# First group of a fused recurrence and two-layer MLP kernel on one Trainium2 core: all first-layer weight loads queued ahead of the decays of group 2, two buffers for the range-check sums, other slots for sums and scans

## The chip, the core and the metric

One core of a Trainium2 chip runs the whole kernel. The metric is the device time of one execution in microseconds. Three runs of the kernel before gave 985.7, 987.65 and 989.75 us, median 987.65. The trace is of one more execution.

## The reference

```
for t in range(768):                        # B=4, H=8, D=48: y is (B,H,S,D)
    y[:, :, t] = r[t] @ (state + outer(u * k[t], v[t]))
    state = w[t][..., None] * state + outer(k[t], v[t])
x = y transposed to (3072 tokens, 384)
h = x @ w_in                                # 384 -> 2048
g = where(h >= 1, h, where(h <= -1, 0, (h + 1)**2 / 4))
x = g @ w_out                               # 2048 -> 384
g2 = x @ w_gate;  v2 = x @ w_val            # 384 -> 1536 each
out = (g2 * sigmoid(g2) * v2) @ w_out2      # 1536 -> 384
```

All in float32. The kernel computes each float32 product as three products of a high and a low part (`hi*hi`, `lo*hi`, `hi*lo`).

## The kernel before

**Tiling.** The 3,072 tokens are eight groups of 384 tokens, a group is three windows of 128. `phase1` goes over the groups and, in each, over 16 slots `j` of the first MLP; `phase2` does the same for the second MLP. In slot `j` TensorE runs `tile_in(j+2)` (nine matmuls of 128x384, L1142) and `tile_out(j)` (nine, L1170). ScalarE and VectorE make the activation between the two: ScalarE `knee` (L761, L763), VectorE `knee` (L1004), ScalarE `hi` (L754, rounds to the high part), VectorE `lo` (L997, the low part). VectorE's slot `j` begins with `lo(j+1)` and `knee(j+2)`.

**The recurrence** of group g+1 is computed in the slots of group g. VectorE scans the decays `w` backwards and forwards (`suffix_scan` L907 and L910, `prefix_scan` L917; both together are `scan_window`), scales `k` and `r` (`scale_window`, L929 and L932), sums the products of one token (`diag_sum`, L937), decays the state (L958), masks the attention tile (L973), adds up the state (L985) and the output of a window (L989), and splits the transposed output (L992). TensorE's pieces of it are called fills: KT (L1185), AT (L1193), ST (L1202), Y (L1210, L1215) and XT (L1221). A fill needs a bank of PSUM that an earlier fill's readers have given back: AT of window 1 needs the banks of Y and ST of window 0, so it waits for L989 and L985. `WIN_SLOTS` puts the fills into slots 3, 5, 6, 8, 9, 11 and 12. GpSimd makes the token products (`diag_products`, L658 and L661) and, from the sums, the values (`diag_values`, L668).

**The first group is special.** Its own recurrence runs before slot 0 with nothing beside it. And in it the weights of the first MLP arrive: 32 chunks `c` of 192 KB, even ones of `w_in`, odd ones of `w_out`. The queue of SyncE loads chunk c into slot c % 13 of a ring, once both parts of chunk c - 13 are made (`load_w1`). ScalarE makes the high part (`w1_hi`, L699), two chunks in each slot; the low part is made by GpSimd (L645) for three chunks of four and by VectorE (`w1_lo`, L1033) for every fourth: 3, 7, 11 up to 31. `tile_in(j)` needs chunk 2j and `tile_out(j)` chunk 2j+1.

**What sets the order.** Every engine and the queue of SyncE go in program order, which is written out by hand. Tables say in which slot of group 0 VectorE and ScalarE do what for group 1: `CHECK_FIRST`, `SCAN_FIRST`, `SCALE_FIRST`, `DIAG_FIRST`, `LO_FIRST`. `PRODUCTS_AT` and `VALUES_AT` say after which chunk GpSimd makes the products and values of a window of group 1. SyncE issues `load_w(2, w)`, the decays of group 2, ahead of the last five weight chunks (27 to 31); each waits until VectorE has scaled the same window of group 1 (`scaled`, L932), because the tile is reused.

**The range check.** ScalarE's `check_w` (L715) sums, over each window, how far `w` lies outside of the range for which the fast scans hold, into the six columns of `beyond`; VectorE's `sum_w` (L943) adds them to `bad`. With one `beyond` the check of the next group may begin only when `sum_w` of the group before is done. A slow exact version behind `If(flagged > 0)` is not taken here.

Of the kernel before, what the change touches and what calls it, by code (L numbers as in the profile page):

```python
# [24 lines left out]
F32 = mybir.dt.float32  # L25
F32R = mybir.dt.float32r
U32 = mybir.dt.uint32
ALU = mybir.AluOpType
# [8 lines left out]
NW = 3  # L37
# [3 lines left out]
PR = 64 + D  # L41
KT = DM // P
J1, J2 = FF1 // P, FF2 // P
# [4 lines left out]
RING = 13  # L48
# [23 lines left out]
OPS_CHECK = 2 * NW  # L72
# [13 lines left out]
CHECK_FIRST = {0: 1, 2: 2}  # L86
SCAN_FIRST = {1: 1, 4: 2}
SCALE_FIRST = {0: 0, 2: 1, 7: 2}
DIAG_FIRST = {2: 0, 4: 1, 6: 2}


DVE_LO = 4
LO_FIRST = {0: 7, 1: 11, 3: 15, 4: 19, 6: 23, 8: 27, 10: 31}
PRODUCTS_AT = {8: 0, 13: 1, 20: 2}
VALUES_AT = {12: 0, 18: 1, 25: 2}


def first(g):
    return isinstance(g, int) and g == 0
# [6 lines left out]
def fill_no(g, kind, w, n=0):  # L106
    return fills(g).index((kind, w, n))


def build_program(nc, w_d, kr_d, tok_d, u_d, cst_d, w1i_d, w1o_d, w2g_d, w2v_d,  # L110
                  w2o_d, rs_d, ks_d, vs_d, ws_d, us_d, out_d, x2_d, ys_d):
    ctx = ExitStack()
    with ctx:
        at = [nc.sbuf_base + (-nc.sbuf_base) % 32]

        def place(name, shape, dt, offset=None):

            size = 2 if dt == mybir.dt.bfloat16 else 4
            for n in shape[1:]:
                size *= n  # L120
            if offset is None:
                offset = at[0]
                at[0] += (size + 31) // 32 * 32
            assert offset + size <= nc.sbuf_usable_end, (name, offset + size)
            return nc.alloc_sbuf_tensor_at(name, shape, dt, offset=offset), offset + size
# [11 lines left out]


        checked, _ = place("w_checked", [PR, NPAIR * WIN], mybir.dt.bfloat16)
        beyond, _ = place("w_beyond", [PR, OPS_CHECK], F32)  # L140
        bad, _ = place("w_bad", [PR, OPS_CHECK + 1], F32)
        ones, _ = place("ones", [PR, 1], F32)

# [359 lines left out]
        def _(e):  # L503
# [13 lines left out]
            def load_w1(n):  # L517

                for c in range(chunk[0], min(chunk[0] + n, 2 * J1)):
                    if c >= RING:  # L520
                        wait(whi, c - RING + 1)
                        wait_lo(wait, c - RING)
                    src = (w1i_d if c % 2 == 0 else w1o_d)[c // 2]
                    e.dma_start(chunk_raw(c), src).then_inc(raw[c % RING], 16)
                chunk[0] += n
# [13 lines left out]
            def load_tok(g, w):  # L539

                if g > 0:
                    wait(fill, (g - 1) * NF + fill_no(g - 1, "ST", w) + 1)
                    wait(y_out, (g - 1) * NW + w + 1)
                e.dma_start(tok[:, w, :, :], tok_d[g, w]).then_inc(ld["tok", w], 16)
# [8 lines left out]
            load_w(0, 2)  # L553
            load_kr(0, 2)
            load_tok(0, 1)
            load_w1(1)
            load_tok(0, 2)
            load_w1(3)
            for w in range(NW):
                load_w(1, w)  # L560
            load_w1(RING - 4)
            for w in range(NW):
                load_kr(1, w)
                load_tok(1, w)
            load_w1(14)
            for w in range(NW):
                load_w(2, w)
            load_w1(2 * J1)

            def half(g, after_next):  # L570

# [123 lines left out]
        def _(e):  # L695
# [5 lines left out]
            def check_w(g, w):  # L701

                if w == 0:
                    if first(g):
                        e.wait_ge(tables, 1)
                    else:
                        e.wait_ge(w_sum, g + 1)
                e.wait_ge(ld["w", w], (g + 1) * 16)
                src = tokens_of(w_at, w)[:, :, 1:]
                junk = checked[:, :].rearrange("q (p t) -> q p t", t=WIN)  # L710
                for k, (scale, bias) in enumerate(((-1.0, W_LOW), (1.0, -W_HIGH))):
                    m = 2 * w + k
                    if not (first(g) and m == 0):
                        e.wait_ge(w_seen, g * OPS_CHECK + m)
                    e.activation(junk, src, ACT.Relu, bias=bias, scale=scale,  # L715
                                 accum_out=beyond[:, m:m + 1]).then_inc(w_seen, 1)

            def decay_first(w):

# [67 lines left out]
            drain(0, fill_no(0, "ST", 0), 0)  # L787
            decay_first(1)
            drain(0, fill_no(0, "KT", 1), 0)
            done = [0]  # L790

            def more_hi(n):
# [10 lines left out]
            drain(0, fill_no(0, "XT", 1), 0)  # L803
            more_hi(8)
            drain(0, fill_no(0, "XT", 2), 0)
            check_w(1, 0)
            more_hi(11)
            knee(0, 0)
            hi(1, 0, 0)
# [88 lines left out]
        def _(e):  # L898
# [41 lines left out]
            def sum_w(g):  # L940
                e.wait_ge(w_seen, (g + 1) * OPS_CHECK)
                e.wait_ge(w_sum, g + 1)
                e.tensor_tensor(bad[:, 0:OPS_CHECK], bad[:, 0:OPS_CHECK], beyond[:, :], ALU.add).then_inc(w_sum, 1)  # L943

            def decay_state(g, w, parity):

# [82 lines left out]
            def w1_lo(c):  # L1029
                t = w1i if c % 2 == 0 else w1o  # L1030
                e.wait_ge(whi, c + 1)
                e.wait_ge(raw[c % RING], 16 * (c // RING + 1))
                e.tensor_tensor(t[1][:, c // 2, :], chunk_raw(c), t[0][:, c // 2, :].bitcast(F32),  # L1033
                                ALU.subtract).then_inc(wlo_d, 1)
# [22 lines left out]
            drain(0, fill_no(0, "XT", 1), 0)  # L1057
            drain(0, fill_no(0, "XT", 2), 0)
            drain(0, fill_no(0, "ST", 2), 0)
            suffix_scan(1, 0)  # L1060
            w1_lo(3)
            prefix_scan(1, 0)
            knee(0, 0)
            lo(1, 0, 0)
            knee(0, 1)

            def nxt(g, j, J_):
                return (g, j) if j < J_ else (g + 1, j - J_)
# [289 lines left out]
```

## Time and profile before

| | |
|---|---|
| three runs, median | 987.65 us (985.7 to 989.75) |
| the profiled execution, its own time | 987.91 us |
| its span, first to last instruction | 986.0 us |
| TensorE busy | 960.7 us, 97% |
| VectorE, ScalarE, GpSimd busy | 522.1, 404.3, 149.6 us |
| mean granted TensorE clock | 0.996 |
| group 0, slot 0 begins at | 35.9 us |
| group 0, slot 15 ends near | 107 us |

The span counts from the first to the last instruction, and what lies around it in this execution is 1.9 us. An engine's busy time counts an instruction from its start to its end, waiting for a shared resource included. An idle time stands in front of the instruction that ended it, with what released it.

### The profile page before, as it was taken

The numbers are of one execution on the slowest core, as the hardware profiler recorded it, in microseconds if no ns is written. First come the engines' busy times: TensorE is split into PE (matmuls) and PEld (weight loads), VectorE is DVE, ScalarE is ACT, GpSimd is POOL, SyncE is SP. The second block draws the span as 40 slices with busy tenths as digits, with TensorE's granted clock in tenths as the row PEclk, the third lists the DMA queues.
The fourth block names the chain that finished last, engine by engine and source line by source line (L and its number), as shares of the span: only waits on it lengthen the run. The fifth ranks groups of instructions, "written<-read, shape, count | busy, mean of one in ns | idle before, by whom it ended". The sixth has DMA issues, their size and how long they took to land.

```text
span 986.0 us, 17455 instructions
## 1 busy us (share of the span) xinstructions
PE 960.7 (97%) x6874; PEld 942.0 (96%) x6874; DVE 522.1 (53%) x913; ACT 404.3 (41%) x849; POOL 149.6 (15%) x146
## 2 busy tenths in 40 slices
PE   5898999999999999999999999999999999999997
PEld 4888999999999999999999999999999999999997
DVE  8895757657576665665434434434343343344332
ACT  5855546445464454544565322222222222222221
POOL 6582120211202102020263300000000000000000
PEclk9998999999999999999999999999999999999999
DMA  7916131321313222100332201010100001010000
GB/s 249 279 34 178 44 96 47 93 77 54 96 44 95 58 73 81 59 25 1 121 105 89 73 1 49 1 49 2 48 0 15 33 0 48 0 48 0 25 1 26
DMA packets 23204, 59.52 MB, mean 60 GB/s; under 512 B 2656, under 2 KB 11616, under 8 KB 23136
## 3 DMA queue, kind: packets, MB, share of 16 engines
q1 hardware_dynamic: 23136, 58.59, 19.0%
q8 instruction: 46, 0.75, 0.3%
q14 instruction: 22, 0.18, 0.1%
HBM read 49.14 MB, written 9.44 MB: 59 GB/s over the span
## 4 chain that ended last, share of the span: by engine, by line
PE 91%; DVE 4%; issue 1%; DMA 1%; ACT 1%; SPq 0%; DVEq 0%; ACTq 0%
PE bank L1142 48%; PE bank L1170 34%; PE bank L1193 3%; PE bank L1215 2%; PE bank L1210 2%; PE bank L1185 1%; PE bank L1221 1%; PE bank L1202 1%; DVE glo L997 1%; DVE suf L907 1%; DVE k_r_by_channel L929 1%; DMA ring<-in_w_gate 1%; DVE gate L1004 1%; DVE k_r_by_channel L932 0%; DVE state_decayed L958 0%
## 5 line engine op out<-in xcount | busy, mean ns | idle before, releaser
L997 DVE TENSOR_TENSOR glo<-gate,ghi 128x384 fp32r<-128x384 f32 x224 | 134.6, 601 | 114.6 <-ACT ghi L754 112.2
L754 ACT ACTIVATE ghi<-gate 128x384 fp32r<-128x384 f32 x224 | 117.2, 523 | 189.9 <-DVE gate L1016 95.4
L1014 DVE TENSOR_TENSOR gate<-bank,gate 128x384 f32<-128x384 f32 x96 | 53.5, 558 | 215.0 <-ACT gate L873 215.0
L1142 PE MATMUL bank<-xhi,w2gv_ahi 128*128 128x384 f32 x480 | 161.3, 336 | 0.0
L1142 PE MATMUL bank<-xlo,w2gv_ahi 128*128 128x384 f32 x480 | 161.3, 336 | 0.0
L1142 PE MATMUL bank<-xhi,w2gv_alo 128*128 128x384 f32 x480 | 161.3, 336 | 0.0
L873 ACT ACTIVATE gate<-bank 128x384 f32<-128x384 f32 x96 | 47.2, 492 | 227.7 <-PE bank L1142 227.7
L1170 PE MATMUL bank<-ghi,w1ohi 128*128 128x384 f32 x384 | 134.6, 350 | 0.3 <-DVE glo L997 0.3
L1142 PE MATMUL bank<-xhi,w1ihi 128*128 128x384 f32 x384 | 129.5, 337 | 4.2 <-DVE gate L1004 1.5
L1170 PE MATMUL bank<-glo,w1ohi 128*128 128x384 f32 x384 | 129.7, 338 | 0.0
L1170 PE MATMUL bank<-ghi,w1olo 128*128 128x384 f32 x384 | 129.6, 337 | 0.0
L1142 PE MATMUL bank<-xhi,w1ilo 128*128 128x384 f32 x384 | 129.2, 336 | 0.0
L1142 PE MATMUL bank<-xlo,w1ihi 128*128 128x384 f32 x384 | 129.1, 336 | 0.0
L1004 DVE SCALAR_TENSOR_TENSOR gate<-bank,gate 128x384 f32<-128x384 f32 x128 | 71.1, 556 | 106.2 <-ACT gate L763 106.1
L761 ACT ACTIVATE gate<-bank 128x384 f32<-128x384 f32 x128 | 62.7, 490 | 90.2 <-PE bank L1142 90.2
L1170 PE MATMUL bank<-ghi,w2ohi 128*128 128x384 f32 x288 | 96.8, 336 | 0.0
L1170 PE MATMUL bank<-ghi,w2olo 128*128 128x384 f32 x288 | 96.8, 336 | 0.0
L1170 PE MATMUL bank<-glo,w2ohi 128*128 128x384 f32 x288 | 96.8, 336 | 0.0
L1142 PEld LDWEIGHTS bank<-xhi,w2gv_ahi 128*128 128x128 f32 x480 | 90.2, 188 | 0.0
L1142 PEld LDWEIGHTS bank<-xlo,w2gv_ahi 128*128 128x128 f32 x480 | 90.2, 188 | 0.0
L1142 PEld LDWEIGHTS bank<-xhi,w2gv_alo 128*128 128x128 f32 x480 | 90.2, 188 | 0.0
L1142 PEld LDWEIGHTS bank<-xhi,w1ihi 128*128 128x128 f32 x384 | 72.3, 188 | 5.0 <-issue 3.2
(90 smaller groups left out, 1530.7 us busy)
## 6 DMA issues: line engine op xcount, KB each, us to landing
r_k_v_by_token<-in_rkv_token SPq DMA_DIRECT2D x24, 576.0 KB, 4.9
k_r_by_channel<-in_kr_channel SPq DMA_DIRECT2D x24, 448.0 KB, 3.9
w_by_channel<-in_w_channel SPq DMA_DIRECT2D x24, 226.2 KB, 2.7
x_t<-ring SPq DMA_DIRECT2D x8, 576.0 KB, 3.0
x_raw<-x_t SPq DMA_DIRECT2D x8, 576.0 KB, 4.0
out_t<-ring SPq DMA_DIRECT2D x8, 576.0 KB, 3.1
ring<-in_w_out SPq DMA_DIRECT2D x22, 192.0 KB, 3.3
ring<-in_w_gate SPq DMA_DIRECT2D x12, 192.0 KB, 2.3
```

Source lines behind the costliest of these rows:

```text
L754: e.activation(ghi[j % 2][:, :], gate[j % 2][:, :], ACT.Copy).then_inc(M["hi", ph], 1)
L761: e.activation(q, hid[j % 2][:, 0:T], ACT.Relu, bias=0.5, scale=0.5).then_inc(M["q", 1], 1)
L873: e.activation(gate[j % 2][:, :], hid[j % 2][:, 0:T], ACT.Sigmoid).then_inc(M["q", 2], 1)
L907: e.tensor_tensor_scan(suf[:, w, ::-1], w_at[:, w, :0:-1], last[:, ::-1], 0.0, ALU.mult, ALU.max).then_inc(scan, 1)
L997: e.tensor_tensor(glo[j % 2][:, :], gate[j % 2][:, :], ghi[j % 2][:, :].bitcast(F32), ALU.subtract)\
L1004: e.scalar_tensor_tensor(q, hid[j % 2][:, 0:T], 1.0, q, ALU.max, ALU.min).then_inc(M["g", 1], 1)
L1014: e.tensor_tensor(q, hid[j % 2][:, 0:T], q, ALU.mult).then_inc(M["t", 2], 1)
L1142: m = e.matmul(out, w_of(a, k), x_of(b_, k), start=start and i == 0, stop=stop and i == total - 1)
L1170: m = e.matmul(acc[k][:, 0:T], wo[a][:, j, k * P:(k + 1) * P], gs[b_][:, :], start=(j == 0 and i == 0), stop=(j == J[ph] - 1 and i == 2))
L1193: m = e.matmul(o[:, p * WIN:(p + 1) * WIN], kr[r, w, 0, p, :], kr[r, w, 1, p, :], start=True, stop=True)
L1210: e.matmul(out[t, p * 2 * D:(p + 1) * 2 * D], kr[:, w, 1, p, t], sbar[twin(g, w)][:, p, :], start=(p == 0), stop=False, skip_group_check=True)
L1215: m = e.matmul(out[t, h * D:(h + 1) * D], att[twin(g, w)][h % 2][:, h // 2, t], tok[:, w, 2, h * D:(h + 1) * D], start=(row_start and h == 0),
```

## The change

1. **SyncE's queue, late.** `load_w(2, w)`, w = 0, 1, 2, goes behind all 32 weight chunks; it stood behind chunk 26.
2. **SyncE's queue, early.** `load_w(1, 0)` goes ahead of chunk 0 and of the tokens of window 2, and chunk 4 goes ahead of `load_w(1, 1)`.
3. **Checks.** `beyond` gets two buffers, one for even and one for odd groups, and `check_w(g, 0)` waits only for the sum of group g-2. ScalarE's `check_w(1, 0)` moves from behind XT of window 2 to behind KT of window 1 of group 0.
4. **VectorE.** `w1_lo(3)` goes ahead of `suffix_scan(1, 0)`, and `prefix_scan(1, 0)` behind `knee(0, 1)`. The `diag_sum`s of group 1 go from slots 2, 4, 6 to 0, 3, 5; chunk 15 goes from slot 3 to 2 and chunk 27 from slot 8 to 9.
5. **GpSimd.** Values of windows 0, 1, 2 behind chunks 13, 19, 26 (before 12, 18, 25), products of window 1 behind chunk 14 (before 13).

```diff
-DIAG_FIRST = {2: 0, 4: 1, 6: 2}
+DIAG_FIRST = {0: 0, 3: 1, 5: 2}
-LO_FIRST = {0: 7, 1: 11, 3: 15, 4: 19, 6: 23, 8: 27, 10: 31}
-PRODUCTS_AT = {8: 0, 13: 1, 20: 2}
-VALUES_AT = {12: 0, 18: 1, 25: 2}
+LO_FIRST = {0: 7, 1: 11, 2: 15, 4: 19, 6: 23, 9: 27, 10: 31}
+PRODUCTS_AT = {8: 0, 14: 1, 20: 2}
+VALUES_AT = {13: 0, 19: 1, 26: 2}
...
-        beyond, _ = place("w_beyond", [PR, OPS_CHECK], F32)
+        beyond, _ = place("w_beyond", [PR, 2, OPS_CHECK], F32)
...
             load_tok(0, 1)
+            load_w(1, 0)
             load_w1(1)
             load_tok(0, 2)
-            load_w1(3)
-            for w in range(NW):
+            load_w1(4)
+            for w in range(1, NW):
                 load_w(1, w)
-            load_w1(RING - 4)
+            load_w1(RING - 5)
...
-            load_w1(14)
+            load_w1(2 * J1)
             for w in range(NW):
                 load_w(2, w)
-            load_w1(2 * J1)
...
                 if w == 0:
-                    if first(g):
-                        e.wait_ge(tables, 1)
-                    else:
-                        e.wait_ge(w_sum, g + 1)
+                    e.wait_ge(tables, 1)
+                    if g > 1:
+                        e.wait_ge(w_sum, g)
...
-                                 accum_out=beyond[:, m:m + 1]).then_inc(w_seen, 1)
+                                 accum_out=beyond[:, g % 2, m:m + 1]).then_inc(w_seen, 1)
...
             drain(0, fill_no(0, "KT", 1), 0)
+            check_w(1, 0)
...
             drain(0, fill_no(0, "XT", 2), 0)
-            check_w(1, 0)
             more_hi(11)
...
             drain(0, fill_no(0, "ST", 2), 0)
+            w1_lo(3)
             suffix_scan(1, 0)
-            w1_lo(3)
-            prefix_scan(1, 0)
             knee(0, 0)
             lo(1, 0, 0)
             knee(0, 1)
+            prefix_scan(1, 0)
```

`sum_w` reads `beyond[:, g % 2, :]` accordingly. Where the rows of the order speak of the changed kernel, its line numbers from ScalarE's part on are one lower.

**SyncE, the end of group 0's weight loads; before:**

```order
L524 DMA ring_b<-in_w_out 128x384
L524 DMA ring<-in_w_in 128x384
L531 DMA w_by_channel<-in_w_channel 112x517 x3
L524 DMA ring<-in_w_out 128x384
L524 DMA ring<-in_w_in 128x384
L524 DMA ring<-in_w_out 128x384
```

and changed:

```order
L524 DMA ring<-in_w_out 128x384
L524 DMA ring<-in_w_in 128x384
L524 DMA ring<-in_w_out 128x384
L531 DMA w_by_channel<-in_w_channel 112x517 x3
L537 DMA k_r_by_channel<-in_kr_channel 112x1024
```

The three loads of decays (L531) stood between chunks 26 and 27; now they stand behind chunk 31 and directly ahead of the `k` and `r` of group 2.

**GpSimd, from chunk 9 on, first where the low parts of chunks 12 to 18 and the products and values of group 1 stand** (L645 is a low part, L658 and L661 the products, L668 the values). What is printed is the difference of the two:

```order
 L645 TENSOR_TENSOR w1olo<-ring_b,w1ohi 128x384
 L645 TENSOR_TENSOR w1ilo<-ring_b,w1ihi 128x384 x2
+L645 TENSOR_TENSOR w1olo<-ring,w1ohi 128x384
 L668 TENSOR_TENSOR r_k_v_by_token<-r_k_v_by_token,diag 128x384
-L645 TENSOR_TENSOR w1olo<-ring,w1ohi 128x384
+L645 TENSOR_TENSOR w1ilo<-ring,w1ihi 128x384
 L658 TENSOR_TENSOR r_k_v_by_token<-r_k_v_by_token 128x384
 L661 TENSOR_TENSOR r_k_v_by_token<-r_k_v_by_token,u_rows 128x384
-L645 TENSOR_TENSOR w1ilo<-ring,w1ihi 128x384 x2
+L645 TENSOR_TENSOR w1ilo<-ring,w1ihi 128x384
```

Chunk 13 now goes ahead of the values of window 0, and chunk 14 ahead of the products of window 1.

**VectorE, slots 0 to 3 of group 0; before, from `scale_window(1, 0)` of slot 0 on:**

```order
L929 TENSOR_TENSOR k_r_by_channel<-k_r_by_channel,suf 112x512
L932 TENSOR_TENSOR k_r_by_channel<-k_r_by_channel,w_by_channel 112x512
L1033 TENSOR_TENSOR w1olo<-ring_b,w1ohi 128x384
L997 TENSOR_TENSOR glo_57<-gate_53,ghi_55 128x384
L1004 SCALAR_TENSOR_TENSOR gate_54<-bank,gate_54 128x384
L907 SCALAR_TENSOR_TENSOR suf<-w_by_channel,last_of_segment 112x516
L910 RECIPROCAL scan_seed<-suf 112x4
L917 SCALAR_TENSOR_TENSOR w_by_channel<-w_by_channel,scan_seed 112x516
```

and changed:

```order
L928 TENSOR_TENSOR k_r_by_channel<-k_r_by_channel,suf 112x512
L931 TENSOR_TENSOR k_r_by_channel<-k_r_by_channel,w_by_channel 112x512
L936 TENSOR_REDUCE diag<-r_k_v_by_token 128x8
L1032 TENSOR_TENSOR w1olo<-ring_b,w1ohi 128x384
L996 TENSOR_TENSOR glo_57<-gate_53,ghi_55 128x384
L1003 SCALAR_TENSOR_TENSOR gate_54<-bank,gate_54 128x384
L906 SCALAR_TENSOR_TENSOR suf<-w_by_channel,last_of_segment 112x516
L909 RECIPROCAL scan_seed<-suf 112x4
L916 SCALAR_TENSOR_TENSOR w_by_channel<-w_by_channel,scan_seed 112x516
```

The sum of window 0 (L936) stands two slots earlier, ahead of chunk 7; the rest of the order is kept there.

## Rows read from the trace of the kernel before

**Rows 1.** Waits of TensorE (engine, line, releaser: us in total, times, longest), 0 to 140 us

```profile
PE bank L1193 <- DVE x_by_token L989: 3.8, 2, 3.0
PE bank L1142 <- DVE gate L1004: 1.5, 1, 1.5
PE bank L1142 <- POOL w1ilo L645: 1.4, 1, 1.4
```

**Rows 2.** Busy time by stretch: PE, PEld, DVE, ACT, POOL, then granted clock, DMA share, GB/s

```profile
42.00:49.50 7.50, 7.50 (x55) 7.20 (x54) 7.36 (x14) 7.09 (x18) 0.00 (x0) 1.00 0.80 258
49.50:62.00 12.50, 11.11 (x117) 10.52 (x116) 12.30 (x17) 6.29 (x14) 12.36 (x10) 1.00 0.20 64
75.00:80.00 5.00, 2.47 (x15) 2.15 (x13) 1.39 (x5) 1.81 (x4) 0.69 (x1) 0.97 0.84 240
80.00:85.00 5.00, 4.57 (x25) 4.38 (x26) 3.94 (x8) 2.17 (x6) 0.95 (x2) 0.50 0.96 258
```

**Rows 3.** Timeline of SyncE's queue: start, us, line, transfer

```profile
52.32 22.15 SPq L531 DMA_DIRECT2D w_by_channel<-in_w_channel  x3
```

**Rows 4.** Timelines of ScalarE and VectorE behind that load; in brackets the idle time

```profile
78.10 0.52 ACT L699 ACTIVATE w1ohi<-ring 128x384 fp32r<-128x384 f32 x1 [3.19 <-DMA ring<-in_w_out]
...
79.59 0.73 DVE L985 TENSOR_TENSOR state<-bank,state_decayed 48x192 f32<-48x192 f32 x2
```

**Rows 5.** Timeline of TensorE: first matmuls of `tile_in` 8, 9, 11, 12; AT of windows 1, 2

```profile
61.10 0.34 PE L1142 MATMUL bank<-xhi,w1ihi 128*128 128x384 f32 x1
...
63.71 1.16 PE L1193 MATMUL bank<-k_r_by_channel 48*128 48x128 f32 x16 [0.89 <-DVE x_by_token L989]
...
66.75 0.34 PE L1142 MATMUL bank<-xhi,w1ihi 128*128 128x384 f32 x1
...
75.75 0.34 PE L1142 MATMUL bank<-xhi,w1ihi 128*128 128x384 f32 x1
...
80.43 2.08 PE L1193 MATMUL bank<-k_r_by_channel 48*128 48x128 f32 x16 [2.96 <-DVE x_by_token L989]
...
86.02 0.52 PE L1142 MATMUL bank<-xhi,w1ihi 128*128 128x384 f32 x1
```

**Rows 6.** Timeline of GpSimd: chunk 12, and the values of window 0 that followed

```profile
40.40 1.33 POOL L645 TENSOR_TENSOR w1ilo<-ring_b,w1ihi 128x384 fp32r<-128x384 f32 x1 [1.03 <-ACT w1ihi L699]
49.56 1.01 POOL L668 TENSOR_TENSOR r_k_v_by_token<-r_k_v_by_token,diag 128x384 f32<-128x384 f32 x1 [7.84 <-DVE diag L937]
```

**Rows 7.** VectorE's groups of instructions, 42.1 to 49.5 us: busy us, mean ns

```profile
L997 DVE TENSOR_TENSOR glo<-gate,ghi 128x384 fp32r<-128x384 f32 x3 | 1.6, 549 | 0.0
...
L907 DVE TENSOR_TENSOR_SCAN suf<-w_by_channel,last_of_segment 112x516 f32<-112x516 f32 x1 | 1.2, 1217 | 0.0
...
L1033 DVE TENSOR_TENSOR w1olo<-ring_b,w1ohi 128x384 fp32r<-128x384 f32 x2 | 1.1, 538 | 0.0
```

**Rows 8.** The same groups of VectorE, 49.5 to 62 us

```profile
L997 DVE TENSOR_TENSOR glo<-gate,ghi 128x384 fp32r<-128x384 f32 x3 | 2.7, 900 | 0.0
L958 DVE TENSOR_TENSOR state_decayed<-state,suf 48x192 f32<-48x192 f32 x2 | 2.2, 1113 | 0.0
L1004 DVE SCALAR_TENSOR_TENSOR gate<-bank,gate 128x384 f32<-128x384 f32 x3 | 1.6, 547 | 0.0
L1033 DVE TENSOR_TENSOR w1olo<-ring,w1ohi 128x384 fp32r<-128x384 f32 x2 | 1.6, 787 | 0.0
L907 DVE TENSOR_TENSOR_SCAN suf<-w_by_channel,last_of_segment 112x516 f32<-112x516 f32 x1 | 1.6, 1569 | 0.0
```

**Rows 9.** Timeline of VectorE: `lo(2)`, `lo(6)`, state of window 0, decay of window 2

```profile
42.67 0.55 DVE L997 TENSOR_TENSOR glo<-gate,ghi 128x384 fp32r<-128x384 f32 x1
...
60.41 1.18 DVE L997 TENSOR_TENSOR glo<-gate,ghi 128x384 fp32r<-128x384 f32 x1
...
62.88 0.73 DVE L985 TENSOR_TENSOR state<-bank,state_decayed 48x192 f32<-48x192 f32 x2
...
81.42 0.73 DVE L958 TENSOR_TENSOR state_decayed<-state,suf 48x192 f32<-48x192 f32 x2
```

More of the change, by code:

```diff
@@ L942, in sum_w @@
                 e.wait_ge(w_sum, g + 1)
-                e.tensor_tensor(bad[:, 0:OPS_CHECK], bad[:, 0:OPS_CHECK], beyond[:, :], ALU.add).then_inc(w_sum, 1)
+                e.tensor_tensor(bad[:, 0:OPS_CHECK], bad[:, 0:OPS_CHECK], beyond[:, g % 2, :], ALU.add).then_inc(w_sum, 1)
             def decay_state(g, w, parity):
```

## The prediction

> **What bounds the kernel now.** The first view is the list of TensorE's waits together with the busy time by stretch. TensorE is busy for 97% of the span, and the waits of any size are in group 0 and at the two ends. In slots 0 to 15 of group 0 it waited four times: twice for the bank of L1193 (0.9 and 3.0 us), 1.5 us for `knee(0, 0)` of VectorE, and 1.4 us for the low part of chunk 14 by GpSimd [rows 1]. The reader should see that the largest wait is one alone, and that the stretch around it is also the only one in which the granted clock is 0.50 [rows 2].
>
> The second view is the timeline of the engines around that wait. SyncE's queue was at the decays of group 2 from 52.32 to 74.47 us, because the last of these waits for L932 of window 2, and chunk 27 stands behind it [rows 3]. ScalarE had come to chunk 27 and idled 3.19 us for its landing, VectorE stood behind ScalarE's high part, and only then came the drains of window 1 (L989, L985), whose banks AT of window 2 needs [rows 4]. TensorE resumed at 80.43 us, after 2.96 us, and its sixteen matmuls of AT then took 2.08 us where those of window 1 took 1.16 [rows 5].
>
> The third view, VectorE's busy time, says what comes next. In 42 to 62 us VectorE was busy for 19.66 of 20 us, and TensorE's wait at 63.7 us ended with VectorE's L985 of window 0 (62.88 + 0.73 us) [rows 2, 5, 9]. So up to the load stall the pace is set by VectorE, with TensorE close behind. And VectorE's time is not all its own: from 42 to 49.5 us GpSimd did nothing and `lo` took 549 ns, a low part of a chunk 538, a suffix scan 1,217; from 49.5 to 62 us GpSimd was busy 12.36 of 12.5 us and the same took 900, 787 and 1,569, the decays of a window 2.2 us for the pair against 0.73 alone. `knee`, which reads a bank, took 547 either way [rows 2, 6 to 9]. I read this as the two engines taking turns at something that instructions with two SBUF inputs need.
>
> **Part 1, the late loads (the gain).** With all 32 chunks ahead of L531, chunk 27 waits only for the low part of chunk 14, and chunk 31 for that of 18, all of which exist before 61 us; the queue was idle then. The stall of ScalarE and VectorE goes. Its price is read as a whole: from `tile_in(11)` to `tile_in(12)` TensorE took 86.02 - 75.75 = 10.27 us. The same work (AT, XT, `tile_out`, `tile_in`) took 66.75 - 61.10 = 5.65 us two windows earlier, 0.89 of it waiting and 0.17 the last matmul running out, so 4.6 without a wait [rows 5]. The stall cost 5.7 us: 3.0 of waiting and 2.7 of half clock. Behind it L531 comes to wait for window 2 of group 1 as before, and the decays, `k` and `r` of group 2 go out right then, where five chunks stood ahead of them: nothing becomes later.
>
> **Part 2, the early loads and the moved check: nothing.** `load_w(1, 0)` and the chunks behind it wait for L932 of window 0, but there transfers are queued up behind one another, so the order of bytes counts and not the moment of issue. 226 KB more ahead of the tokens of window 2 is 0.9 us at the 258 GB/s of another full stretch [rows 2], and GpSimd comes to those tokens late. ScalarE's check falls into an idle stretch ahead of KT of window 2. If that cover were gone, its 1.5 us would stand ahead of that drain; where it was, ScalarE now is free 1.4 us earlier, ahead of `knee(0, 0)`.
>
> **Part 3, the prefix scan and the two first waits: nothing in the end.** `knee(0, 0)` no longer stands behind a scan, and TensorE's 1.5 us go. But what was moved (1.2 us of scan) and the sum of window 0 (0.5 us) are now ahead of slot 1, so VectorE reaches `lo(2)` at about 42.6 us, as before (42.67) [rows 1, 9]. The wait for chunk 14 (1.4 us) goes too, since GpSimd no longer idles ahead of it. Both gains are swallowed at the next point where TensorE catches up with VectorE.
>
> **Part 4, GpSimd's turns (the loss).** Before, GpSimd idled 7.84 us for the sum of window 0 [rows 6], and these were VectorE's undisturbed slots. Now the sum is done ahead of slot 1 and GpSimd runs on: chunk 13, values, chunk 14, products (two), chunks 16, 17, 18, of which none ran before 49.5 us before. In slots 1 to 3 VectorE has its longest strings of two-input instructions (two scans, chunk 11, `lo(3)`; then L929, L932, chunk 15, `lo(4)`), and behind each of them a waiting GpSimd gets its turn. I count up to `lo(6)`. Before, from 42.67 to 60.41 + 1.18 = 61.59 us, VectorE took 18.9 us. Of these the excess over undisturbed was 3 x 0.35 (`lo`) + 1.5 (decays) + 2 x 0.25 (chunks) + 2 x 0.35 (scans) = 3.75 us, for 9 instructions of GpSimd: 0.42 each [rows 7 to 9]. Own work is 15.2 us, now 14.7 without the sum. Against it stand 14 instructions of GpSimd (5 more: chunks 20, 21, 22 and the two products of window 2). A turn costs between 0 (VectorE is at a `knee`, sum or bank copy) and GpSimd's 0.9. Going through the strings in order I get about 7.3 us, 0.52 each, since more of them fall into strings. So `lo(6)` ends at 42.6 + 14.7 + 7.3 = 64.6 us, 3.0 later. The sum of window 2 now also stands ahead of L989 (+0.5), while `sum_w`'s turn (0.4) falls away. VectorE gives back the banks 3 us later, and TensorE, whose later waits were all behind that point, is 3.0 us later until 77 us. Bounds: at the old 0.42 a turn 5.9 us, so 1.7 us late; at 0.62 8.7 us, so 4.5 late. I take 3.0 because most of the added turns are in strings.
>
> **The sum.** 987.9 (the profiled execution) - 5.7 + 3.0 = 985.2 us; with the bounds 983.9 and 986.7. The profiled execution lies 0.26 us above the median of the runs, so the two can be compared as they are. A measurement of this kernel can tell about 0.5% (4.9 us) from no change, so 985.2 is within.
>
> **The clock, weighed.** TensorE's waits of 0.9 to 1.5 us left the granted clock at 1.00; the one of 2.96 us was followed by 0.50 [rows 1, 2, 5]. In the sum above TensorE waits at AT of window 1 from about 63.5 to 66.8 us, which is as long. The Trainium skill ("TensorE: Matmul & The Clock Gate", Part 1) says that the array's clock is halved by default, that activity releases it and idleness brings the half clock back, at a moment that shifts from run to run. By that rule the stretch of half clock would only move from 80 to 67 us, and the sum would be 2.7 us more, 987.9; by the clock as it stands elsewhere in the trace it is 985.2.
>
> **The rivals.**
> - *The half clock moves along.* If VectorE is 3 us late in one piece, TensorE has one wait of some 3 us again, and the clock falls as it did at 80 us. 987.9 - 5.7 + 3.0 + 2.7 = 987.9; from 3.0 us of lateness on it is slower than before, with 4.5 us 989.4. For it: the 2.96 us wait did this. Against it: part of the lateness comes out earlier as waits at `tile_out(2)` and `tile_out(3)`, each under 2.5 us. The page named above has this rule.
> - *Turns cost little.* GpSimd's instructions are only moved, not added, and what it does before 55 us it does not do in 60 to 72 us, where VectorE could catch up. Then lateness is 0 to 1.7 us, and the time 982.2 to 983.9. Against it: at the wait of 63.7 us nothing has been given back yet.
> - *VectorE is not what holds TensorE.* All waits go, 1.5, 1.4 and 0.9 us and 0.17 each of run-out besides the 5.7: 978. Against it: VectorE's 19.66 of 20 us.
> - *A new stall.* `load_w(1, 0)` holds up SyncE's queue for 2 us at the start, or an early chunk or the tokens come late, and the first group's own recurrence, where nothing is beside TensorE, is longer by that much; only with more than 10 us is it slower by 0.5%.
> - *The loads go out no earlier*, because the ring is full: only if chunks 14 to 18 were late, and they had been made by 61 us.
>
> **How the numbers follow.** The sum with the clock held, lateness 1.7 to 4.5 us: 0.42, around 985.2. The half clock moves along: 0.24, 986.6 to 989.4. Turns cost little: 0.20, 982.2 to 983.9. VectorE does not hold TensorE: 0.08, 977 to 981. Anything slower by over 0.5%: 0.04; the rest, 0.02, is spread. The range of 981.8 to 989.0 us leaves out the fourth case, the fifth and the ends of the second. Faster by over 0.5% (under 982.7) are the fourth case, half of the third and a little of the first: 0.22. Slower (above 992.6): 0.04. Within: 0.74.
>
> **What would show it.** Right: no wait of ScalarE or VectorE for a load of `ring` near 75 us, and L531 of group 2 behind the last L524; GpSimd's wait for L937 near 42 us gone; `lo` in 43 to 53 us at 900 ns or more; the state of window 0 (L984 there) near 66 us instead of 62.9; TensorE waiting 2 to 3.5 us for AT of window 1 and for nothing behind it in group 0. Wrong: `lo` stays near 550 ns in 43 to 50 us, or the state of window 0 comes by 63 us; then the gain is the whole 5.7 us or more. The granted clock near 67 us decides between the first two cases.

## The result, and the profile after

The changed kernel takes **997.55 us** (median of 4 runs, 996.58 to 999.85) where the kernel before takes 987.86 us (median of 4, 985.7 to 989.75): a ratio of 1.0106, with a 95% interval of 1.009 to 1.0123. It is slower by 1%, 10 us, where 985.2 us was forecast. The profiled execution took 997.93 us, its span 996.1 us.

The first view is again that of TensorE's waits, of the changed kernel from 0 to 120 us.

```profile
PE bank L1192 <- DVE x_by_token L988: 3.6, 1, 3.6
```

The waits for `knee(0, 0)` and for chunk 14 [rows 1] are gone, and so is the stall at 77.5 us. One long wait stands for them, 3.6 us, for the bank that VectorE hands back; beside it are three short ones for `lo`, 1.9 us together. TensorE's timeline shows where it is, and SyncE's what became of the queue:

```profile
66.28 1.70 PE L1192 MATMUL bank<-k_r_by_channel 48*128 48x128 f32 x16 [3.58 <-DVE x_by_token L988]
```

```profile
56.91 0.33 SPq L524 DMA_DIRECT2D ring<-in_w_out  x1
57.30 20.22 SPq L531 DMA_DIRECT2D w_by_channel<-in_w_channel  x3
```

The last chunk leaves at 56.91 us and L531 of group 2 stands behind it, until 77.52 us, and nobody waits for it. VectorE's timeline beside [rows 9], `lo(2)`, `lo(3)`, `lo(6)` and the state of window 0:

```profile
42.72 1.35 DVE L996 TENSOR_TENSOR glo<-gate,ghi 128x384 fp32r<-128x384 f32 x1
...
48.12 1.35 DVE L996 TENSOR_TENSOR glo<-gate,ghi 128x384 fp32r<-128x384 f32 x1
...
61.86 1.36 DVE L996 TENSOR_TENSOR glo<-gate,ghi 128x384 fp32r<-128x384 f32 x1
...
65.45 0.73 DVE L984 TENSOR_TENSOR state<-bank,state_decayed 48x192 f32<-48x192 f32 x2
```

`lo(2)` starts at 42.72 us (before 42.67), and `lo(6)` ends at 63.22 us, 1.6 later than before. The state comes at 65.45 us instead of 62.88. In GpSimd's timeline the 7.84 us of idling before the values of window 0 [rows 6] are filled:

```profile
43.82 1.12 POOL L645 TENSOR_TENSOR w1olo<-ring,w1ohi 128x384 fp32r<-128x384 f32 x1 [0.16 <-ACT w1ohi L699]
44.90 1.76 POOL L668 TENSOR_TENSOR r_k_v_by_token<-r_k_v_by_token,diag 128x384 f32<-128x384 f32 x1
```

So far this is the forecast in kind and in order; how the sizes compare stands further down. SyncE's store L582 that closes group 0 is issued at 107.81 us where it was issued at 109.22: the reordered stretch is **1.4 us shorter** in these two executions. The 10 us are lost behind it, where the change moves nothing. The busy time by stretch for 100 us in the middle of the program, first before and then after; the list of after begins with the 5 us behind the long wait (columns as in [rows 2]):

```profile
610.00:710.00 100.00, 100.00 (x579) 100.00 (x578) 39.69 (x69) 25.34 (x50) 0.00 (x0) 1.00 0.07 23
```

```profile
65.00:70.00 5.00, 3.72 (x24) 3.53 (x25) 2.48 (x7) 1.34 (x4) 0.03 (x1) 0.67 0.01 3
610.00:710.00 100.00, 100.00 (x570) 100.00 (x570) 38.25 (x67) 24.25 (x46) 0.00 (x0) 1.00 0.04 13
```

The two rows for 610 to 710 us are the ones to read first: TensorE is busy all the time and at the full clock in both kernels, but gets through 570 matmuls instead of 579. The costliest groups of the profile's pages say the same; of before, and of after:

```profile
L1142 PE MATMUL bank<-xhi,w2gv_ahi 128*128 128x384 f32 x480 | 161.3, 336 | 0.0
```

```profile
L1141 PE MATMUL bank<-xhi,w2gv_ahi 128*128 128x384 f32 x480 | 162.1, 338 | 0.0
```

Matmuls overlap, so the number that counts is the time from one start to the next. Averaged over the timeline from 600 to 760 us it was 173.3 ns before and 176.0 ns after, for `xhi` and `xlo` as for `ghi` and `glo`. The trace has 2,880 such matmuls on L1141 and 2,016 on L1169; 4,896 x 2.7 ns = 13.2 us, 12.4 of them behind group 0. The two traces show 11.5 there (10.1 of span and the 1.4 won ahead of it); the 0.9 us between was not traced. The loss is even: each of the 68 strings of nine matmuls between 600 and 760 us took 1.56 us before, and each of the 67 after took 1.58 or 1.59 us. So it does not come and go with what the other engines do at a moment. What the reader is to see: a loss of 1.6% in a loop that the change doesn't touch, at full clock and with no wait, does not look like an order of work. Runs 1 and 2 test that.

**What else the diff does.** `beyond` with two buffers is 48 bytes a partition instead of 24, and `place` rounds to 32. Everything placed behind it, `w_bad`, `ones` and all weights, starts 32 bytes later: the weights at 0 modulo 128 where they stood at 96. The moving operands of the matmuls (`xhi`, `xlo`, `ghi`, `glo`), placed ahead of `beyond`, start at 0 modulo 128 in both. (All places are counted from the start of `xhi` in the kernel of before.) The first theory, P, was that this sets the pace; its rivals were that the order of work does it (O), or the chip or moment (C).

### The profile page after: what moved, and what is told of

It is laid out like the page before. It is cut to its first block, busy times and chain, and to the rows that moved or that the text cites. A ratio compares the mean times of both kernels' runs of the same rounds, so it can differ in the third digit from the quotient of the medians.

```text
span 996.1 us, 17461 instructions
## 1 busy us (share of the span) xinstructions
PE 972.0 (98%) x6874; PEld 953.2 (96%) x6874; DVE 523.9 (53%) x913; ACT 405.0 (41%) x849; POOL 155.4 (16%) x146
## 4 chain that ended last, share of the span: by engine, by line
PE 94%; DVE 4%; issue 1%; ACT 0%; DMA 0%; DVEq 0%; ACTq 0%
PE bank L1141 49%; PE bank L1169 35%; PE bank L1192 2%; PE bank L1214 2%; PE bank L1209 2%; PE bank L1184 1%; PE bank L1220 1%; PE bank L1201 1%; DVE suf L906 1%; DVE glo L996 1%; DVE k_r_by_channel L928 0%; DVE k_r_by_channel L931 0%; DVE gate L1003 0%; DMA w_by_channel<-in_w_channel 0%; DVE att L972 0%
## 5 line engine op out<-in xcount | busy, mean ns | idle before, releaser
L1141 PE MATMUL bank<-xhi,w2gv_alo 128*128 128x384 f32 x480 | 162.1, 338 | 0.0
L1141 PE MATMUL bank<-xlo,w2gv_ahi 128*128 128x384 f32 x480 | 162.1, 338 | 0.0
L1141 PE MATMUL bank<-xhi,w2gv_ahi 128*128 128x384 f32 x480 | 162.1, 338 | 0.0
L1169 PE MATMUL bank<-ghi,w1ohi 128*128 128x384 f32 x384 | 134.8, 351 | 2.0 <-DVE glo L996 1.9
L1141 PE MATMUL bank<-xhi,w1ihi 128*128 128x384 f32 x384 | 130.0, 338 | 1.5 <-issue 1.4
L1169 PE MATMUL bank<-glo,w1ohi 128*128 128x384 f32 x384 | 130.0, 338 | 0.0
L1169 PE MATMUL bank<-ghi,w1olo 128*128 128x384 f32 x384 | 129.9, 338 | 0.0
L1141 PE MATMUL bank<-xhi,w1ilo 128*128 128x384 f32 x384 | 129.7, 338 | 0.0
L1141 PE MATMUL bank<-xlo,w1ihi 128*128 128x384 f32 x384 | 129.7, 338 | 0.0
L1169 PE MATMUL bank<-ghi,w2ohi 128*128 128x384 f32 x288 | 97.3, 338 | 0.0
L1169 PE MATMUL bank<-glo,w2ohi 128*128 128x384 f32 x288 | 97.3, 338 | 0.0
L1169 PE MATMUL bank<-ghi,w2olo 128*128 128x384 f32 x288 | 97.3, 338 | 0.0
L1141 PEld LDWEIGHTS bank<-xlo,w2gv_ahi 128*128 128x128 f32 x480 | 90.1, 188 | 0.0
L1141 PEld LDWEIGHTS bank<-xhi,w2gv_ahi 128*128 128x128 f32 x480 | 90.1, 188 | 0.0
L1141 PEld LDWEIGHTS bank<-xhi,w2gv_alo 128*128 128x128 f32 x480 | 90.1, 188 | 0.0
L668 POOL TENSOR_TENSOR r_k_v_by_token<-r_k_v_by_token,diag 128x384 f32<-128x384 f32 x24 | 28.6, 1193 | 311.6 <-DVE diag L936 311.6
```

The source lines that it names most:

```text
L668: e.tensor_tensor(tok[:, w, 0, :].rearrange("p (h d) -> p h d", d=D), tok[:, w, 2, :].rearrange("p (h d) -> p h d", d=D), d_b, ALU.mult).t ...
L1141: m = e.matmul(out, w_of(a, k), x_of(b_, k), start=start and i == 0, stop=stop and i == total - 1)
L1169: m = e.matmul(acc[k][:, 0:T], wo[a][:, j, k * P:(k + 1) * P], gs[b_][:, :], start=(j == 0 and i == 0), stop=(j == J[ph] - 1 and i == 2))
```

## Four runs on the place of the weights

**Run 1.** Before, with 32 bytes ahead of the weights and nothing else.

```
         ones, _ = place("ones", [PR, 1], F32)
+        pad, _ = place("pad", [PR, 8], F32)
```

> The kernel before, with nothing changed but 32 unused bytes on each partition between `ones` and the weights: every weight tile and everything behind it starts 32 bytes later, as in the changed kernel. Theory P (the place of the weights): the matmuls of 128x384 take 175.5 ns from start to start instead of 173.3, as in the changed kernel, and the time is 987.9 + 4,896 x 2.2 ns = 998 to 999 us, the changed kernel's 997.6 plus what that gains in group 0. Rival O (the order of work, more turns of GpSimd or the queue): no change, 988 us, 173.3 ns. Rival C (another chip or another moment has a slower array): the kernel before would be slower in this job too, and the two stay the same.

Measured: 1001.03 us, ratio 1.0125 (1.0107 to 1.0144), 176.0 ns from start to start. The kernel of before is made slower than the changed one by 32 unused bytes. Its row for the stretch:

```profile
610.00:710.00 100.00, 100.00 (x570) 100.00 (x570) 38.13 (x67) 24.27 (x47) 0.00 (x0) 1.00 0.04 13
```

**Run 2.** The changed kernel with the weights back at their old place: `ones` becomes a column of `bad`.

```
-        bad, _ = place("w_bad", [PR, OPS_CHECK + 1], F32)
-        ones, _ = place("ones", [PR, 1], F32)
+        bad, _ = place("w_bad", [PR, OPS_CHECK + 2], F32)
+        ones = bad[:, OPS_CHECK + 1:OPS_CHECK + 2]
...
```

The places where `ones` and `bad` are used are changed to match.

> The changed kernel, with `ones` in the last four bytes of the 32 that `w_bad` takes up, so that the second buffer of `w_beyond` takes its place and all weights start where they did before the change. Theory P: 173.3 ns a matmul and 997.6 - 10.8 = 986.5 us, a little under the kernel before, by what group 0 gains (slot 15 ends 1.4 us earlier). Rival O: 997 us, as the changed kernel. Rival C: 997 us beside a kernel before that is slower too.

Measured: 985.77 us (8 runs), ratio 0.9974 (0.9962 to 0.9985), 579 matmuls in the stretch. With its own order of work and the old place, the change comes within 0.6 us of the time that was forecast for it, 985.2. O and C fall. The store that closes group 0 is at 107.66 us, TensorE's wait at AT of window 1 is 3.6 us. Its row for the stretch:

```profile
610.00:710.00 100.00, 100.00 (x579) 100.00 (x578) 39.14 (x68) 25.39 (x49) 0.00 (x0) 1.00 0.07 24
```

**Runs 3 and 4.** As run 1, with 64 and 96 bytes (`[PR, 16]` and `[PR, 24]`): weights at 32 and at 64 modulo 128.

> The kernel before with 64 unused bytes ahead of the weights. Theory P leaves open what it is in the place that counts. If only the start modulo 64 bytes counts, this is the kernel before: 988 us and 173.3 ns. If it is the start modulo 128 (96 before, 0 in the changed kernel, 32 here), it may be either. Rival O: 988 us.

> The kernel before with 96 unused bytes ahead of the weights, so that they start at 64 modulo 128. If the start modulo 64 counts, this is as the pad of 32 bytes: 998 us and 175.5 ns. If only a start at 0 modulo 128 is slow, 988 us. Rival O: 988 us.

Measured: 1003.39 us (ratio 1.0143, 1.0123 to 1.0163; 176.7 ns) for 64 bytes, 988.64 us (1.0002, 0.9988 to 1.0017; 173.3 ns) for 96. So weights at 64 and 96 are fast, at 0 and 32 slow. The two expectations had left it open which of the places would be slow.

## Place by itself, or against the moving operands

**Run 5.** All tiles from `xhi` on 64 bytes later. **Run 6.** The same, and the weights 32 bytes more.

```
+        ahead, _ = place("ahead", [PR, 16], F32)
         xhi = [place(f"xhi{i}", [P, KT, T], F32R)[0] for i in range(2)]
```

```
         ones, _ = place("ones", [PR, 1], F32)
+        pad, _ = place("pad", [PR, 8], F32)
```

The second piece is in run 6 alone.

> The kernel of before with 64 bytes put ahead of xhi, so that everything from the moving operands on starts 64 bytes later: the moving operands (xhi, xlo, gate, ghi, glo) at 64 modulo 128 where they stood at 0, the weights at 32 modulo 128 where they stood at 96. The distance between the two is as before. Theory 'absolute': what counts is where the weights start modulo 128 by itself, so this is slow like the run with 64 bytes ahead of the weights: about 1003 us, 176.5 ns from one matmul of 384 columns to the next. Rival 'relative': what counts is where the weights start against the moving operands; then it is as before, about 988 us and 173.3 ns.

> 64 bytes ahead of xhi and 32 more ahead of the weights: moving operands and weights both start at 64 modulo 128. Theory 'absolute': the weights at 64 are fast, so about 988 us and 173.3 ns a matmul, as in the run with 96 bytes ahead of the weights. Rival 'relative': the distance is 0 as in the changed kernel, so about 1001 us and 176 ns.

Measured: 988.7 us (ratio 1.0013, 1.0004 to 1.0022; 173.3 ns) for run 5, 1000.39 us (1.0141, 1.0125 to 1.0156; 176.0 ns) for run 6. The place by itself, which I favoured, falls: weights at 32 modulo 128 were slow in run 3 and are fast here, where the moving operands moved with them. It is the distance from what stands ahead of them.

**Run 7.** The changed kernel, weights where it puts them, but the moving operands 32 bytes up; the weights are kept in place by run 2's diff. The distance is 96 as before the change.

```
+        ahead, _ = place("ahead", [PR, 8], F32)
         xhi = [place(f"xhi{i}", [P, KT, T], F32R)[0] for i in range(2)]
```

> The changed kernel with its weights where it has them (0 modulo 128), the moving operands moved 32 bytes up instead (to 32 modulo 128, distance 96 as before the change); the place for the weights is kept by putting ones into w_bad's bytes. Theory 'relative': fast, 173.3 ns a matmul, 985.5 us. Rival: the start of the weights by itself, 997.5 us.

Measured: 986.95 us (12 runs), ratio 0.9988 (0.9974 to 1.0002), 579 matmuls in the stretch. The weights start at 0 modulo 128 as in the slow kernel, and it is fast:

```profile
610.00:710.00 100.00, 100.00 (x579) 100.00 (x578) 38.86 (x68) 24.99 (x48) 0.00 (x0) 1.00 0.07 24
```

| moving operands at | weights at | runs | ns from start to start |
|---|---|---|---|
| 0, 64, 32 | 96, 32, 0 (distance 96) | before and run 2; 5; 7 | 173.3 |
| 0 | 64 (distance 64) | 4 | 173.3 |
| 0, 64 | 0, 64 (distance 0) | after and run 1; 6 | 176.0 |
| 0 | 32 (distance 32) | 3 | 176.7 |

(All modulo 128 bytes.) Distances 32 and 64 were measured at one place of the moving operands each. And the runs move blocks of tiles: `gate`, the ring and the constants go with the moving operands, the tiles of the recurrence with the weights. That the operands of TensorE are what counts is an argument, from an engine that waits for nobody and is slowed in every matmul alike; no run moves them alone.

**Runs 8 to 10: whose distance?** If a matmul's pace went by its own moving operand, shifting `ghi` and `glo` alone would split the two kinds. Run 8 puts 32 bytes between `gate` and `ghi`; run 9 96 there and 32 ahead of the weights; run 10 32 there and 96 ahead of the weights. The diff is that of run 8; in run 9 the 8 is 24, and `pad` of runs 1 and 4 comes with 9 and 10.

```
+        apart, _ = place("apart", [P, 8], F32)
         ghi = [place(f"ghi{i}", [P, T], F32R)[0] for i in range(2)]
```

> The kernel of before with 32 bytes between gate and ghi/glo: xhi and xlo start at 0 modulo 128, ghi, glo and the weights 32 bytes later than before, at 32 and at 0. Theory 'relative': the pace of a matmul goes by where its weights start against its own moving operand. Then the matmuls of the first layer's kind (weights 0, moving xhi or xlo 0: distance 0) are slow, 175.9 ns apart and 338 in the row, and those of ghi and glo (weights 0, moving 32: distance 96 as before) stay fast, 173.3 and 336. Of the 4,896 matmuls 2,880 have xhi or xlo as moving operand: 2,880 x 2.6 = 7.4 us more than before, about 994.7 us. Rival 'weights or other tiles alone': all of them are slow (1,001 us) or none (988).

> The kernel of before with 96 bytes between gate and ghi and 32 ahead of the weights: xhi and xlo at 0 modulo 128, weights at 96 (distance 96 as before), ghi and glo at 96 (distance 0). Theory 'own moving operand': the 2,880 matmuls of xhi and xlo are fast (173.3 ns apart), the 2,016 of ghi and glo slow (176): 2,016 x 2.6 = 5.2 us more than before, about 993 us. Rival 'more than the own operand' (from the mixed answer for ghi and glo): the two sorts pull one another, and all of them lie between, at any time from 988 to 1001 us.

> 32 bytes between gate and ghi and 96 ahead of the weights: xhi and xlo at 0, weights at 96 (distance 96), ghi and glo at 32 (distance 64, which was fast for all in the run with 96 bytes ahead of the weights). Theory 'own moving operand': all fast, 173.3 ns and 988 us. Rival: that ghi stands 32 bytes off xhi costs by itself, and this is slower than 988 by up to 5 us, with the matmuls of ghi and glo at 175 ns as in the first run that moved them.

| run | `xhi`, `xlo`: distance, ns | `ghi`, `glo`: distance, ns | time, ratio (95%) |
|---|---|---|---|
| 8 | 0, 176.2 | 96, 175.0 | 997.36, 1.0088 (1.0063 to 1.0113) |
| 9 | 96, 175.0 | 0, 175.6 | 995.73, 1.0086 (1.0069 to 1.0103) |
| 10 | 96, 176.6 | 64, 172.6 | 997.28, 1.0098 (1.0081 to 1.0115) |

The rule of the own operand fails, and with it the forecasts for runs 8 and 10; run 9 came out as its rival had it, with `xhi` and `xlo` at 175.0 ns instead of 173.3. Run 10 is the clearest: both distances were fast in the runs above, and the kernel is 10 us slower. Its groups show one kind at 335 to 336 ns and the other at 338 to 339; the ends of the two:

```profile
L1144 PE MATMUL bank<-xlo,w2gv_ahi 128*128 128x384 f32 x480 | 162.5, 339 | 0.0
...
L1172 PE MATMUL bank<-ghi,w2ohi 128*128 128x384 f32 x288 | 96.4, 335 | 0.0
```

More than one distance matters, and the three runs in which the two kinds of moving operand stand apart are all slow. In what way the places act on the matmuls stays open: I have a table of places, not a mechanism.

## The order of work, with the pace held

**Run 11.** Before, with the late loads alone; weights at their old place.

```
-            load_w1(14)
+            load_w1(2 * J1)
             for w in range(NW):
                 load_w(2, w)
-            load_w1(2 * J1)
```

> The kernel of before with nothing but the last five chunks put ahead of the decays of group 2; weights where they were. Theory (Part 1 of the prediction): the stall at 77.5 to 80.4 us goes with its half clock, and nothing else changes: 5.7 us less, 982 us. GpSimd's places are as before, so the state of window 0 comes near 62.9 us as before and no wait of TensorE in group 0 is over 2 us. Rival 1: another wait takes the place of the stall, so that only the 2.7 us of half clock or less is won: 985 to 988. Rival 2: the half clock is not tied to the stall and stays somewhere in 62 to 85 us: 985.

Measured: 983.17 us against 987.1 in the same session, ratio 0.996 (0.9947 to 0.9974), a gain of 3.9 us by the medians and 4.7 by the spans. TensorE's timeline has the two first matmuls of `tile_in` 11 and 12, and AT of window 2 between them without a wait, at full clock:

```profile
76.98 0.34 PE L1141 MATMUL bank<-xhi,w1ihi 128*128 128x384 f32 x1
...
78.64 1.16 PE L1192 MATMUL bank<-k_r_by_channel 48*128 48x128 f32 x16
...
81.68 0.34 PE L1141 MATMUL bank<-xhi,w1ihi 128*128 128x384 f32 x1
```

They are 4.70 us apart where they were 10.27 us apart [rows 5]: the stall cost 5.57 us, against 5.7 in the sum. By the spans the kernel gains less, 4.7 us, because this execution lost 1.2 us before slot 0. TensorE's Y fill of 32 matmuls started there at 24.67 us in the trace of before and at 24.54 us in run 11, and took 1.27 and 1.89 us; the XT fill behind it took 0.55 and 0.90 us. The lengths are those of the half clock (an AT fill just ahead took 2.08 us in both, as at 0.50 in [rows 5]), though the column of the granted clock reads 1.00 in both stretches.

Run 11 is 0.13 us ahead at 24.6 us and 1.2 us behind at the first matmul of `tile_in(0)` (32.25 us against 31.05), and stays so until the stall's place. The moment at which the matmuls become fast differs from execution to execution, and is worth 1 us here.

**Run 12.** Run 2 (the changed kernel, weights at the old place) with the four tables of before; late loads, moved check and moved scan stay.

```
-DIAG_FIRST = {0: 0, 3: 1, 5: 2}
+DIAG_FIRST = {2: 0, 4: 1, 6: 2}
-LO_FIRST = {0: 7, 1: 11, 2: 15, 4: 19, 6: 23, 9: 27, 10: 31}
-PRODUCTS_AT = {8: 0, 14: 1, 20: 2}
-VALUES_AT = {13: 0, 19: 1, 26: 2}
+LO_FIRST = {0: 7, 1: 11, 3: 15, 4: 19, 6: 23, 8: 27, 10: 31}
+PRODUCTS_AT = {8: 0, 13: 1, 20: 2}
+VALUES_AT = {12: 0, 18: 1, 25: 2}
```

> The changed kernel with the weights at their old place (as in the second run) and with the five numbers of the tables for group 0 (decay diagonals, low parts, products, values) as in the kernel of before; late loads, the moved check and the moved scan stay. Theory 'GpSimd's turns' (Part 4): with fewer instructions of GpSimd set among VectorE's strings ahead of lo(6), VectorE comes earlier to the state of window 0 than at 65.45 us, and TensorE's wait of 3.6 us at AT of window 1 shrinks: 982 to 984 us. Rival: the turns come from the moved check and sum, with which GpSimd runs on from 42 us, and not from the tables: then the wait stays at 3 us or more and the time at 985.8 us.

Measured: **981.76 us**, ratio 0.9956 (0.9943 to 0.997), the fastest kernel of the study. The state of window 0 starts at 62.18 us, and TensorE does not wait at AT of window 1 (0.9 us in run 13). The wait that is left is for chunk 14, 2.5 us here and 1.7 in run 13. TensorE's waits from 40 to 110 us:

```profile
PE bank L1141 <- POOL w1ilo L645: 2.5, 1, 2.5
```

**Run 13** is run 12 again, beside run 7 on one chip, since runs 2 and 12 were measured apart.

> The run with the old tables once more, beside the changed order with the same distance of weights and moving operands (the second run of this job), to measure the two against each other on one chip. Theory: what stood between them, 4 us, stays: 981.8 against 985.8 us. Rival: part of that lay between the two jobs, and it is 2 us or less.

Measured: 982.03 us, ratio 0.9932 (0.9913 to 0.9951), and 4.9 us under run 7's 986.95 in the same session (spans 980.1 and 983.7; the closing store of group 0 at 102.90 and 107.12 us). The tables of the change cost 4 to 5 us, and the store shows them lost within group 0. The tables were changed together; which entry costs what was not measured.

**Run 14.** Run 12 with GpSimd's wait taken from TensorE's path: values of window 0 and products of window 1 behind chunk 14.

```
-PRODUCTS_AT = {8: 0, 13: 1, 20: 2}
-VALUES_AT = {12: 0, 18: 1, 25: 2}
+PRODUCTS_AT = {8: 0, 15: 1, 20: 2}
+VALUES_AT = {14: 0, 18: 1, 25: 2}
```

> The run with the old tables, with the products of window 1 and the values of window 0 put behind chunk 14 on GpSimd, so that TensorE's 2.5 us wait for the low part of chunk 14 goes. Theory (VectorE is what bounds 42 to 62 us): two more turns of GpSimd stand ahead of VectorE's strings, 0.5 us each, and TensorE, earlier by 2.5 us and 0.8 of half clock, waits for VectorE's state of window 0 instead, some 3 us; the time stays within 1 us of the old tables (981.8), on either side. Rival: TensorE's wait for GpSimd was the bound, and 2.5 to 3.3 us are won: 978.5 to 979.5.

Measured: 985.19 us, ratio 0.9962 (0.9947 to 0.9976), 3.2 us slower than run 13 beside it. The wait for chunk 14 is gone, and the same wait for VectorE as in the changed kernel is back, with the half clock behind it. From TensorE's timeline and from the busy time by stretch:

```profile
65.06 1.47 PE L1192 MATMUL bank<-k_r_by_channel 48*128 48x128 f32 x16 [3.15 <-DVE x_by_token L988]
```

```profile
65.00:70.00 5.00, 4.94 (x30) 4.75 (x31) 3.91 (x6) 1.40 (x4) 4.29 (x4) 0.66 0.02 3
```

TensorE waits for VectorE as expected, but the time is 3.2 us longer where at most 1 us either way was forecast. The two traces tell where it lies. The state of window 0 starts at 64.23 us, 1.9 later than in run 13 (62.37), but `lo(2)` already starts 1.35 us later (43.51 against 42.16 us), ahead of the instructions that were moved; 0.9 of this lies before slot 0. From `lo(2)` to the state VectorE takes 20.72 us instead of 20.21, so the moved instructions cost it 0.5 us and not the 1.0 that I had counted. The half clock behind the wait costs 1.5 us: from AT of window 1 to the fourth matmul of `tile_in` TensorE takes 5.11 us (65.06 to 70.17) instead of 3.57 (63.20 to 66.77). The 1.35 us that the two executions differ by at `lo(2)` are not explained by the edit, though the two sets of runs do not overlap (984.75 to 985.45 and 981.35 to 983.24). So removing the wait for GpSimd won nothing; how much of the 3.2 us is VectorE's time is open.

## Why the prediction was wrong

**The step that failed** is in the list of what the change does. The prediction went through loads, check, scan and turns; the second buffer of `beyond` was put at nothing by not being costed. It named no effect of it, and none of the rivals had it. What the runs showed in its place: the 32 bytes slow every matmul of 384 columns from 173.3 to 176.0 ns, and 4,896 x 2.7 ns are some 13 us. This term alone carries the result out of the range: 985.77 (run 2, the same order of work without the 32 bytes) lies in it, 997.55 does not. Nor was there a row of before to price it from, since a trace at one set of places does not show another; it could only have been named as an unknown, by asking of every changed size what it moves.

**Part 1, the late loads:** right. 5.57 us by run 11 against 5.7, and no wait behind L531 appeared in its place.

**Parts 2 and 3:** right as far as they can be seen. Both first waits went, `lo(2)` started at 42.72 us against the 42.6 foreseen, and the gains were gone by the next hand-back. No run has them alone. The closing store of run 12, which has them, is 1.35 us ahead of that of run 11, which has not (103.30 and 104.65); these are single executions, and the spread before slot 0 is as large.

**Part 4, GpSimd's turns:** right in kind and place, but the sizes were off one by one. `lo(6)` ended 1.6 us late instead of 3.0, which is the lower bound of the sum (0.42 us a turn). Then `sum_w`, whose turn the sum had as 0.4 us saved, took 0.98 us (64.07 us) where it took 0.51 before, and with the sum of window 2 ahead of it the state of window 0 came 2.6 us late. TensorE's wait of 3.6 us lay at AT of window 1 as foreseen, and nothing of 1 us or more waited behind it in group 0. The half clock behind that wait, which the sum left out, cost 1.6 us more: from AT of window 1 to the fourth matmul of `tile_in` 5.13 us in the changed kernel and 3.57 in run 13. The whole is some 4 us where the sum had 3.0.

**Luck.** That run 2 came within 0.6 us of 985.2 is in part luck: the turns were too dear in the sum and the half clock was missing from it. By the medians of its session run 2 gains 2.5 us, by the spans of the two executions 1.6; 2.7 was forecast.

**The half clock** fell again, so that was the rival "the half clock moves along" (0.24), in mild form: run 2's 985.77 us lies below its 986.6 to 989.4. After the 3.58 us wait the granted clock was 0.67 in 65 to 70 us, and TensorE was slow until 70.2 us; before it was slow through the whole of 80 to 85 us (0.50). The prediction took the length of the wait for the condition. The runs show that the length alone does not decide. In run 12 the matmuls became slow (0.52 us each from 55.80 us) after a wait of 2.46 us, in run 4 after 2.25 us. In run 9 they became slow after 2.10 us and stayed fast after 2.29 us. Its TensorE timeline and its busy time by stretch:

```profile
56.62 0.41 PE L1144 MATMUL bank<-xhi,w1ihi 128*128 128x384 f32 x1 [2.10 <-POOL w1ilo L647]
...
81.90 1.16 PE L1195 MATMUL bank<-k_r_by_channel 48*128 48x128 f32 x16 [2.29 <-DVE x_by_token L991]
```

```profile
58.00:60.00 2.00, 2.00 (x11) 1.56 (x12) 1.97 (x3) 0.92 (x2) 2.00 (x2) 0.50 0.00 0
82.00:86.00 4.00, 4.00 (x34) 3.88 (x35) 3.85 (x7) 3.08 (x8) 1.89 (x3) 1.00 0.92 238
```

The moment differs too: in runs 2 and 7, after waits of 3.64 and 3.66 us, AT of window 1 still ran at full speed (1.16 us), and the granted clock was 0.50 in 68 to 70 us.

**The rivals** "VectorE is not what holds TensorE" and "a new stall" fell. "Turns cost little" fell in the changed kernel: the state of window 0 came 2.6 us late, where it allowed 1.7, though `lo(6)` alone, 1.6 us late, lay within it.

## What to carry to other kernels

Ask of each edit what it moves in memory, not only in time: a size in the middle of a list of placements moves all that is behind it, and a second buffer of 24 bytes for a scratch tile cost 1% of a kernel that is bound by TensorE. When a loop that nothing touched changes its pace at full clock and without a wait, pad the old kernel by the same bytes before looking at the schedule. Placing the operands of TensorE ahead of the scratch tiles would keep later edits from moving them; that was not tried here. And where two engines slow one another, the idle time of one can be of use to the other: before filling it, see whether the others wait for the busy one.

## What the runs showed of the hardware

- The pace of this kernel's matmuls of 384 columns, streaming back to back at full clock, goes with where the weights and the moving operands start in SBUF modulo 128 bytes, each with the tiles that move along: 173.3 ns at a distance of 64 or 96 bytes with all moving operands alike (runs 2, 4, 5, 7), 176.0 at 0 (runs 1, 6), 176.7 at 32 (run 3), and 172.6 to 176.6 by kind with two sorts of moving operands at different places (runs 8 to 10).
- The Trainium skill ("TensorE: Matmul & The Clock Gate", Back-to-back issue gap) gives columns / 2.4 GHz + 2.5 ns as the gap of a single matmul by itself, which is an estimate of 162.5 ns for 384 columns, and says that streams of weight loads and matmuls have other spacings. The matmuls here are such a stream, and no arrangement here averaged under 173.3 ns.
- TensorE's granted clock fell to 0.50 after waits of 2.10 us (run 9) and 2.96 us [rows 5], and stayed at 1.00 after one of 2.29 us (run 9).
- VectorE and GpSimd hold one another up. `lo` took 549 ns with GpSimd idle and 1.35 us in the changed kernel (42.72 us), and a low part on GpSimd took 1.0 to 2.4 us. The Trainium skill ("GPSIMD Engine Reference", Specifications) names the shared way to SBUF for VectorE's instructions with two SBUF inputs; the trace agrees, since the fused product of `knee`, which reads a bank, took 0.55 us throughout.
